# VectorE's order in a three-tap convolution loop: both outer taps ahead of an earlier chunk's product, in a fused three-network kernel

## The chip, the cores and the metric

The kernel runs on one core of one Trainium2 chip. The metric is the device time of one execution in microseconds (us), as the median of several runs. TensorE does matrix products, ScalarE activations and copies, VectorE elementwise work, GpSimd some small arithmetic, and SyncE issues the transfers.

## The reference, cut to what matters

Three networks run one after the other in float32. The first is an attention with features that are products of two sketches, the second a Fourier mixing with a normalised two-layer network, the third a network with a convolution of three taps along the sequence. The change is in the third:

```python
def _moe2_ref(x, w_in, conv_w, w_out):          # x: 4 x 1088 x 128, w_in: 128 x 1024
    h = np.maximum(x @ w_in, 0.0)
    hp = ...                                     # h with one row of zeros at either end
    conv_out = np.zeros_like(h)
    for k in range(3):
        conv_out += conv_w[k][None, None, :] * hp[:, k:k + S, :]
    gate = 1.0 / (1.0 + np.exp(-conv_out))
    return (h * gate @ w_out).astype(np.float32)
```

## The kernel before, in words

The last network's tiles lie in SBUF with the channels on the 128 partitions and the tokens along the free dimension. The last network is cut into NI = 32 chunks: chunk i is batch i // 8 and hidden channels (i % 8) * 128 and the following 127, over all 1088 tokens. There is no scheduler. Each engine's program is written out by hand and engines wait for each other through counting semaphores, so the order in the code is the order on the engine.

One chunk i passes through these steps:

- TensorE, `hidden(i, t)`: the hidden values in three pieces of 364 tokens, each as three matmuls (L519, L520, L521) of high and low parts.
- ScalarE, `relu(i)` (L790): three pieces into `h2`, a ring of HIDDENS = 5 tiles. It waits until the product of chunk i - 5, the last reader of its tile, is done.
- ScalarE, `middle_tap(i)` (L798): the middle tap times `h2` into `gate`, a ring of GATES = 9 tiles, from chunk 3 on. For the first three chunks VectorE does this (`opening_tap`, L1034).
- VectorE, `left_tap(i)` (L1043) and `right_tap(i)` (L1048): each adds its tap times shifted `h2` to `gate`, in place. The right tap waits for `left_ready`, the left tap's semaphore.
- ScalarE, `sigmoid(i)` (L803), in place, released by the right tap.
- VectorE, `product(i)` (L1055): `h2` times `gate`, in place. The last two chunks are done in three pieces each, one after the other.
- TensorE, `project(i)` (L598): three pieces, accumulated over the 8 chunks of a batch; each leaves two records in the trace, so six a chunk. After a batch's last chunk ScalarE copies the sums (L811) and SyncE stores them.

TensorE's loop does `hidden(i)`, then pieces of the second network that are left (`slots_a`, L519 to L521, and L559), then the projections of chunks 6 to 8 behind (`LAGS`), of 4 behind from chunk 30 on. After the last hidden matmuls it does the projections of chunks 27 to 31 in a row. ScalarE's loop does `relu(i + 1)`, `middle_tap(i + 1)`, `sigmoid(i - 1)`. VectorE's loop does left tap i, product i - 2 and right tap i, with low parts of the second network's results (L982, L969) in between at a few places, where `slots_a` and `slots_b` have any.

All of these tiles except TensorE's inputs lie in one large tensor, `arena`, so most rows name that tensor.

Of the kernel before, what the change touches and what calls it, by code (L numbers as in the profile page):

```python
# [70 lines left out]
NI = B * (D2 // 128)  # L71
# [39 lines left out]
def build(nc, kT_d, qT_d, v_d, s_d, ident_d, chan_d, cos_d, sin_d, w1_d, w2_d, win_d, wout_d, cw_d, out_d):  # L111
    with ExitStack() as ctx:
# [157 lines left out]
        def has_low(n):  # L270
            return n < LOW_UNTIL
# [30 lines left out]
        def token_views(x2, r):  # L302
            for side in range(2):
                turned = ps[:, bank_x2(r), side * BP * TQ:(side + 1) * BP * TQ]
                (_, b0, j0), (_, b1, j1) = UNITS[r][side * BP:(side + 1) * BP]
                if b0 != b1:
                    rows, (_, columns) = token_range(j0, side)
                    yield turned.rearrange("p (b t) -> p b t", t=TQ)[:, :, rows], x2[:, b0:b1 + 1, columns]
                elif side == 1:
                    for k in range(2):  # L310
                        rows, (_, columns) = token_range(j0 + k, side)
                        yield turned[:, k * TQ + rows.start:k * TQ + rows.stop], x2[:, b0, columns]
                else:
                    first, step = (1, 1) if j0 in LOW else (1 + S // 2, -1)
                    yield (turned.rearrange("p (j t) -> p t j", t=TQ),
                           x2[:, b0, first:first + step * 2 * TQ:step].rearrange("p (t j) -> p t j", j=2))

        def slots_a(i):
            return range(slots_before(2 * i), slots_before(2 * i + 1))

        def slots_b(i):
            return range(slots_before(2 * i + 1), slots_before(2 * i + 2))
# [519 lines left out]
        def _(dve):  # L842
# [91 lines left out]
            def mixed_rows(r):  # L934

                q, j = divmod(r, NJ)
                dve.wait_ge(cosine_done, r + 1)
                dve.wait_ge(sine_ready, r + 1)
                if r >= 1:
                    dve.wait_ge(u_ready, 4 * r)  # L940
                cosine = ps[0:TQ, SUM_BANK, 0:NS].rearrange("p (b l) -> p b l", l=L)
                for k, op in ((0, ALU.subtract), (1, ALU.add)):
                    dve.tensor_tensor(spec[:, k], cosine, sine[:], op).then_inc(spec_ready, 1)
                dve.wait_ge(spec_ready, 2 * (r + 1))
                for side in range(2):
                    for half_ in range(2):
                        x = x_nat[:, q * BP:(q + 1) * BP, side * NJ + j, half_ * 64:half_ * 64 + 64]
                        dve.tensor_tensor(x, x, spec[:, side ^ half_, :, half_:half_ + 64], ALU.add).then_inc(u_ready, 1)

            def moments(r):  # L950
                dve.wait_ge(u_ready, 4 * ROWS_OF[r])
                if r >= 1:
                    dve.wait_ge(mv_ready, r)
                for m, u in enumerate(normalised(TURN_ORDER[r])):
                    ins = dve.bn_stats(stats[:, m, :], u)
                ins.then_inc(stats_ready, 1)
                dve.wait_ge(stats_ready, r + 1)
                if r >= 3:
                    dve.wait_ge(rstd_ready, r - 2)
                for m in range(2 * BP):  # L960
                    ins = dve.bn_aggr(mv[:, r % 3, m, :], stats[:, m, :])
                ins.then_inc(mv_ready, 1)

            def normed_low(r):
                dve.wait_ge(unhi_ready, r + 1)
                if 2 <= r < RING:
                    dve.wait_ge(w1_done, C1 * (r - 1))
                high, low = turned(r)
                dve.tensor_tensor(low, ps[:, bank_turned(r), 0:G1], high.bitcast(F32),  # L969
                                  ALU.subtract).then_inc(unlo_ready, 1)  # L970

            def hidden_low(n):
                dve.wait_ge(h1hi_ready, n + 1)
                if n >= 3:
                    dve.wait_ge(w2_done, n - 2)
                dve.scalar_tensor_tensor(out=h1lo[:, n % 3, :], in0=ps[:, bank_h1(n), 0:G1], scalar=0.0,  # L976
                                         in1=h1hi[:, n % 3, :].bitcast(F32), op0=ALU.max, op1=ALU.subtract).then_inc(h1lo_ready, 1)

            def mixed_low(r):
                dve.wait_ge(x2hi_ready, written(r))  # L980
                for (turned, tokens), (_, high) in zip(token_views(x2lo, r), token_views(x2hi, r)):
                    dve.tensor_tensor(tokens, turned, high.bitcast(F32), ALU.subtract).then_inc(x2lo_ready, 1)  # L982

            def slot(n):
                r, c = divmod(n, C1)
                if n < NC1 and has_low(n):
                    hidden_low(n)
                if n in MIXED_AT:
                    mixed_rows(MIXED_AT[n])
                if c == 1 and r >= NJ:  # L990
                    mixed_low(r - 1)
                if n in MOMENTS_AT:
                    moments(MOMENTS_AT[n])
                if c == 2 and 1 <= r < NJ:
                    mixed_low(r - 1)
                if n in TURNS_AT:
                    normed_low(TURNS_AT[n])
# [39 lines left out]
            def left_tap(i):  # L1037
                if i < OPENING:
                    opening_tap(i)
                    dve.wait_ge(opening_ready, i + 1)  # L1040
                else:
                    dve.wait_ge(mid_ready, i - OPENING + 1)
                dve.scalar_tensor_tensor(out=gate[:, i % GATES, 1:S + 1], in0=h2[:, i % HIDDENS, 0:S], scalar=taps[:, i % C2, 0:1],  # L1043
                                         in1=gate[:, i % GATES, 1:S + 1], op0=ALU.mult, op1=ALU.add).then_inc(left_ready, 1)

            def right_tap(i):
                dve.wait_ge(left_ready, i + 1)
                dve.scalar_tensor_tensor(out=gate[:, i % GATES, 1:S + 1], in0=h2[:, i % HIDDENS, 2:S + 2], scalar=taps[:, i % C2, 2:3],  # L1048
                                         in1=gate[:, i % GATES, 1:S + 1], op0=ALU.mult, op1=ALU.add).then_inc(conv_ready, 1)

            def product(i):
                dve.wait_ge(gate_ready, i + 1)
                cuts = [1 + t * TT for t in range(NT)] if i >= SPLIT_FROM else [1]
                for a, z in zip(cuts, cuts[1:] + [S + 1]):
                    dve.tensor_tensor(gate[:, i % GATES, a:z], h2[:, i % HIDDENS, a:z], gate[:, i % GATES, a:z],  # L1055
                                      ALU.mult).then_inc(prod_ready, 1)
# [6 lines left out]
            for i in range(NI + 2):  # L1063
                if i < NI:
                    left_tap(i)
                if i + 1 == LAST_TURN:
                    normed_low(NR - 1)
                for n in slots_a(i + 1):
                    slot(n)
                if i >= 2:  # L1070
                    product(i - 2)
                if i < NI:
                    right_tap(i)
                for n in slots_b(i + 1):
                    slot(n)

# [93 lines left out]
```

## Time and profile before

| what | before |
|---|---|
| median of 3 runs | 259.62 us (259.18, 259.62 and 291.54) |
| profiled execution, its own time | 258.77 us |
| span of the profiled execution | 256.9 us |
| TensorE matmuls busy | 247.5 us, 96% |
| VectorE busy | 221.8 us, 86% |
| ScalarE busy | 183.8 us, 72% |
| TensorE's granted clock | 1.00 |

The span is that of the instructions on the core; the execution's own time is 1.87 us longer. Busy times overlap, so they don't add up. The chunk loop of the last network runs from about 119 us to the end. Starts are counted from the start of the span. On VectorE an instruction may start before the record of the one ahead has ended, so what one takes of the engine is read from start to start.

### The profile page before, as it was taken

How to read it: one execution, taken by the hardware profiler on the slowest of the kernel's cores; microseconds unless marked ns; L12 is line 12 of the kernel's file. 1: busy time of each engine (PE TensorE's matmuls, PEld its weight loads, DVE VectorE, ACT ScalarE, POOL GpSimd, SP SyncE). 2: the span in 40 equal slices, each digit the busy share in tenths (PEclk: the TensorE clock that was granted, in tenths of full speed). 3: DMA queues.
4: the chain of work that ended last, by engine and by line, in shares of the span. 5: the costliest groups of instructions: out<-in, count | busy, mean ns of one | idle time of the engine just before them, and what ended most of it. 6: DMA issues, size and time to landing. Idle time of an engine off the chain costs nothing.

```text
span 256.9 us, 4304 instructions
## 1 busy us (share of the span) xinstructions
PE 247.5 (96%) x1522; PEld 210.2 (82%) x1522; DVE 221.8 (86%) x395; ACT 183.8 (72%) x354; POOL 26.5 (10%) x90
## 2 busy tenths in 40 slices
PE   8999999989999999989999999999999999999985
PEld 7999998989989999878876878787778777787752
DVE  0846978997998779897999999989979999998992
ACT  2342427333486455878999998979999999978872
POOL 0000000002603333474000000000000000000000
PEclk9999999999999999999999999999999999999999
DMA  7959630300000000000000000002000002002002
GB/s 235 396 181 378 268 97 1 95 4 0 3 0 3 1 1 3 0 3 3 0 0 3 0 0 0 3 1 87 0 0 3 0 0 88 3 1 87 0 0 87
DMA packets 4341, 13.04 MB, mean 51 GB/s; under 512 B 736, under 2 KB 1504, under 8 KB 4320
## 3 DMA queue, kind: packets, MB, share of 16 engines
q1 hardware_dynamic: 4176, 12.74, 13.5%
q8 instruction: 12, 0.20, 0.3%
q14 instruction: 9, 0.07, 0.1%
q10 hardware_dynamic: 144, 0.03, 0.1%
HBM read 10.54 MB, written 2.23 MB: 50 GB/s over the span
## 4 chain that ended last, share of the span: by engine, by line
PE 48%; ACT 5%; issue 1%; DVE 1%; ACTq 0%
PE ps L598 22%; PE ps L519 7%; PE ps L521 7%; PE ps L520 7%; PE ps L559 5%; ACT arena L790 1%; ACT arena L803 1%; ACT arena L720 1%; ACT arena L798 1%; DVE arena L1043 1%; DVE arena L1055 0%; PE ps L529 0%; PE ps L550 0%; ACT x2hi L739 0%; ACT arena L811 0%
## 5 line engine op out<-in xcount | busy, mean ns | idle before, releaser
L598 PE MATMUL ps<-arena,wout 128*128 128x364 f32 (+1 forms) x192 | 62.8, 468 | 0.7 <-DVE arena L1055 0.7
L598 PEld LDWEIGHTS ps<-arena,wout 128*128 128x128 f32 x192 | 35.9, 189 | 20.8 <-issue 2.8
L790 ACT ACTIVATE arena<-ps 128x364 f32<-128x364 f32 x96 | 41.1, 491 | 4.5 <-PE ps L521 4.0
L1043 DVE SCALAR_TENSOR_TENSOR arena<-arena,taps 128x1088 f32<-128x1088 f32 x32 | 43.2, 1351 | 0.3 <-ACT arena L798 0.2
L1048 DVE SCALAR_TENSOR_TENSOR arena<-arena,taps 128x1088 f32<-128x1088 f32 x32 | 43.2, 1351 | 0.1
L1055 DVE TENSOR_TENSOR arena<-arena 128x1088 f32<-128x1088 f32 (+2 forms) x36 | 41.5, 1164 | 1.4 <-ACT arena L803 1.2
L519 PE MATMUL ps<-x2hi,wlo 128*128 128x364 f32 x96 | 39.4, 411 | 0.9 <-ACT arena L790 0.7
L803 ACT ACTIVATE arena<-arena 128x1088 f32<-128x1088 f32 x32 | 35.8, 1121 | 1.9 <-DVE arena L1048 1.9
L798 ACT ACTIVATE arena<-arena,taps 128x1088 f32<-128x1088 f32 x29 | 35.4, 1221 | 0.6
L520 PE MATMUL ps<-x2lo,whi 128*128 128x364 f32 x96 | 31.5, 328 | 0.0
L521 PE MATMUL ps<-x2hi,whi 128*128 128x364 f32 x96 | 31.5, 328 | 0.0
L848 DVE TENSOR_TENSOR arena<-arena 109x1280 f32<-109x1280 f32 (+1 forms) x12 | 21.9, 1843 | 6.1 <-ACT arena L671 6.0
L519 PEld LDWEIGHTS ps<-x2hi,wlo 128*128 128x128 f32 x96 | 18.0, 188 | 6.8 <-ACT arena L790 3.2
L520 PEld LDWEIGHTS ps<-x2lo,whi 128*128 128x128 f32 x96 | 18.1, 188 | 3.3 <-issue 1.2
L671 ACT ACTIVATE arena<-ps 109x320 f32<-109x320 f32 (+2 forms) x16 | 6.7, 425 | 18.0 <-PE ps L434 15.6
L446 PE MATMUL ps<-arena 121*128 121x66 f32 x144 | 18.6, 270 | 0.0
L720 ACT ACTIVATE arena<-x_nat,arena 109x128 f32<-109x128 f32 x40 | 16.4, 483 | 2.6 <-POOL arena L402 2.6
L976 DVE SCALAR_TENSOR_TENSOR h1lo<-ps,h1hi 128x436 fp32r<-128x436 f32 x22 | 13.3, 605 | 5.5 <-ACT h1hi L734 5.5
L521 PEld LDWEIGHTS ps<-x2hi,whi 128*128 128x128 f32 x96 | 18.1, 188 | 0.0
L446 PEld LDWEIGHTS ps<-arena 121*128 121x128 f32 x144 | 17.7, 192 | 0.0
L679 ACT ACTIVATE arena<-ps 128x436 f32<-128x436 f32 x20 | 10.6, 536 | 9.3 <-PE ps L461 9.1
L477 PE MATMUL ps<-arena 128*109 128x66 f32 x160 | 17.1, 260 | 0.1
(90 smaller groups left out, 425.4 us busy)
## 6 DMA issues: line engine op xcount, KB each, us to landing
arena<-v_d SPq DMA_DIRECT2D x4, 594.0 KB, 3.8
arena<-qT_d SPq DMA_DIRECT2D x3, 545.0 KB, 6.3
arena<-kT_d SPq DMA_DIRECT2D x3, 544.5 KB, 5.4
out_d<-arena SPq DMA_DIRECT2D x3, 544.0 KB, 2.7
cos_t<-cos_d SPq DMA_DIRECT2D x1, 926.5 KB, 5.8
sin_t<-sin_d SPq DMA_DIRECT2D x1, 926.5 KB, 7.6
arena<-qT_d SPq DMA_DIRECT2D x2, 272.5 KB, 4.2
wraw<-w_d SPq DMA_DIRECT2D x2, 256.0 KB, 5.2
```

The source lines that it names most:

```text
L446: mm = pe.matmul(ps[:, KV_BANK, pair * 2 * V1:(pair + 1) * 2 * V1], kphi[:, b % 2, t, 2 * pair:2 * pair + 2, :].rearrange("p h f -> p (h f)"),
L519: pe.matmul(out, lo, rhi, start=first, stop=False)
L520: pe.matmul(out, hi, rlo, start=False, stop=False)
L521: return pe.matmul(out, hi, rhi, start=False, stop=last)
L598: pe.matmul(ps[:, OUT_BANK + t, 0:z - a], wout[:, c, :], gate[:, i % GATES, a:z], start=(c == 0), stop=(c == C2 - 1)).then_inc(wout_done, 1)
L790: act.activation(h2[:, i % HIDDENS, t * TT:(t + 1) * TT], ps[:, bank_p(n), 0:TT], ACT.Relu).then_inc(h2_ready, 1)
L798: act.activation(gate[:, i % GATES, 1:S + 1], h2[:, i % HIDDENS, 1:S + 1], ACT.Copy, scale=taps[:, i % C2, 1:2]).then_inc(mid_ready, 1)
L803: act.activation(gate[:, i % GATES, 1:S + 1], gate[:, i % GATES, 1:S + 1], ACT.Sigmoid).then_inc(gate_ready, 1)
L848: dve.tensor_tensor(phi.rearrange("p t h (i j) -> p (t h) i j", j=R), a, c, ALU.mult).then_inc(ready, 1)
L1043: dve.scalar_tensor_tensor(out=gate[:, i % GATES, 1:S + 1], in0=h2[:, i % HIDDENS, 0:S], scalar=taps[:, i % C2, 0:1], in1=gate[:, i % GATE ...
L1048: dve.scalar_tensor_tensor(out=gate[:, i % GATES, 1:S + 1], in0=h2[:, i % HIDDENS, 2:S + 2], scalar=taps[:, i % C2, 2:3], in1=gate[:, i % ...
L1055: dve.tensor_tensor(gate[:, i % GATES, a:z], h2[:, i % HIDDENS, a:z], gate[:, i % GATES, a:z], ALU.mult).then_inc(prod_ready, 1)
```

## The change

In every pass of VectorE's loop `right_tap(i)` comes directly behind the left tap (and behind what the second network still has there), and `product(i - 2)` behind both. The other engines' programs are the same, and so are all waits and tiles.

```diff
                 for n in slots_a(i + 1):
                     slot(n)
+                if i < NI:
+                    right_tap(i)
                 if i >= 2:
                     product(i - 2)
-                if i < NI:
-                    right_tap(i)
                 for n in slots_b(i + 1):
                     slot(n)
```

VectorE, the passes of chunks 2 and 3, before. L1043 is a left tap, L1055 a product (of chunks 0 and 1 here), L1048 a right tap, L969 a low part of the second network; `arena` holds `gate` and `h2`:

```order
L1043 SCALAR_TENSOR_TENSOR arena<-arena,taps 128x1088 [waits opening_ready]
L969 TENSOR_TENSOR late_lo<-ps,late_hi 128x436 [waits unhi_ready]
L1055 TENSOR_TENSOR arena<-arena 128x1088 [waits gate_ready]
L1048 SCALAR_TENSOR_TENSOR arena<-arena,taps 128x1088 [waits left_ready]
L1043 SCALAR_TENSOR_TENSOR arena<-arena,taps 128x1088 [waits mid_ready]
L1055 TENSOR_TENSOR arena<-arena 128x1088 [waits gate_ready]
L1048 SCALAR_TENSOR_TENSOR arena<-arena,taps 128x1088 [waits left_ready]
```

The same place with the change:

```order
L1043 SCALAR_TENSOR_TENSOR arena<-arena,taps 128x1088 [waits opening_ready]
L969 TENSOR_TENSOR late_lo<-ps,late_hi 128x436 [waits unhi_ready]
L1048 SCALAR_TENSOR_TENSOR arena<-arena,taps 128x1088 [waits left_ready]
L1055 TENSOR_TENSOR arena<-arena 128x1088 [waits gate_ready]
L1043 SCALAR_TENSOR_TENSOR arena<-arena,taps 128x1088 [waits mid_ready]
L1048 SCALAR_TENSOR_TENSOR arena<-arena,taps 128x1088 [waits left_ready]
L1055 TENSOR_TENSOR arena<-arena 128x1088 [waits gate_ready]
```

The right tap of chunk 2 still has L969 between itself and its left tap; that of chunk 3, as most behind it, follows its left tap directly.

VectorE at the end of the program, the last two passes with taps (chunks 30 and 31, products 28 and 29) and then product 30 in three pieces, before:

```order
L1043 SCALAR_TENSOR_TENSOR arena<-arena,taps 128x1088 [waits mid_ready]
L1055 TENSOR_TENSOR arena<-arena 128x1088 [waits gate_ready]
L1048 SCALAR_TENSOR_TENSOR arena<-arena,taps 128x1088 [waits left_ready]
L1043 SCALAR_TENSOR_TENSOR arena<-arena,taps 128x1088 [waits mid_ready]
L1055 TENSOR_TENSOR arena<-arena 128x1088 [waits gate_ready]
L1048 SCALAR_TENSOR_TENSOR arena<-arena,taps 128x1088 [waits left_ready]
L1055 TENSOR_TENSOR arena<-arena 128x364 [waits gate_ready]
L1055 TENSOR_TENSOR arena<-arena 128x364
L1055 TENSOR_TENSOR arena<-arena 128x360
```

The same place with the change:

```order
L1043 SCALAR_TENSOR_TENSOR arena<-arena,taps 128x1088 [waits mid_ready]
L1048 SCALAR_TENSOR_TENSOR arena<-arena,taps 128x1088 [waits left_ready]
L1055 TENSOR_TENSOR arena<-arena 128x1088 [waits gate_ready]
L1043 SCALAR_TENSOR_TENSOR arena<-arena,taps 128x1088 [waits mid_ready]
L1048 SCALAR_TENSOR_TENSOR arena<-arena,taps 128x1088 [waits left_ready]
L1055 TENSOR_TENSOR arena<-arena 128x1088 [waits gate_ready]
L1055 TENSOR_TENSOR arena<-arena 128x364 [waits gate_ready]
L1055 TENSOR_TENSOR arena<-arena 128x364
L1055 TENSOR_TENSOR arena<-arena 128x360
```

Product 29 was the last but one of the full-length instructions, ahead of the right tap of chunk 31; now it is the last, behind it. Product 31's three pieces follow in both.

## Rows read from the trace of the kernel before

**Rows 1.** The page: busy us, share of the span, instructions of each engine.

```profile
PE 247.5 (96%) x1522; PEld 210.2 (82%) x1522; DVE 221.8 (86%) x395; ACT 183.8 (72%) x354; POOL 26.5 (10%) x90
```

**Rows 2.** Busy time by stage; behind it granted clock, DMA share, GB/s.

```profile
core 0: us, PE busy (x) PEld busy (x) DVE busy (x) ACT busy (x) POOL busy (x), PEclk, DMA share, GB/s
138.00:248.00 110.00, 109.65 (x477) 83.11 (x475) 105.41 (x94) 101.78 (x165) 0.00 (x0) 1.00 0.04 16
248.00:257.00 9.00, 5.76 (x18) 3.32 (x18) 4.27 (x8) 2.54 (x4) 0.00 (x0) 1.00 0.17 62
```

**Rows 3.** The chain that ended last, from 242 us: start us, us, what.

```profile
243.03 0.48 ACT arena L790
...
244.53 1.21 ACT arena L798
...
245.77 1.35 DVE arena L1043
247.12 1.21 DVE arena L1055
...
248.38 5.78 PE ps L598 x18
```

**Rows 4.** Timeline of TensorE at the end; in brackets idle time before, and releaser.

```profile
245.66 2.00 PE L598 MATMUL ps<-arena,wout 128*128 128x364 f32 x6
...
248.38 5.76 PE L598 MATMUL ps<-arena,wout 128*128 128x364 f32 x18 [0.72 <-DVE arena L1055]
```

**Rows 5.** Timeline of VectorE at the end.

```profile
235.56 1.29 DVE L1055 TENSOR_TENSOR arena<-arena 128x1088 f32<-128x1088 f32 x1 [1.24 <-ACT arena L803]
...
238.03 1.35 DVE L1043 SCALAR_TENSOR_TENSOR arena<-arena,taps 128x1088 f32<-128x1088 f32 x1
...
249.50 2.77 DVE L1055 TENSOR_TENSOR arena<-arena 128x364 f32<-128x364 f32 x6
```

**Rows 6.** Timeline of ScalarE: a ReLU, a middle tap, the last sigmoid.

```profile
146.67 1.18 ACT L790 ACTIVATE arena<-ps 128x364 f32<-128x364 f32 x3
...
236.65 1.21 ACT L798 ACTIVATE arena<-arena,taps 128x1088 f32<-128x1088 f32 x1
...
249.62 1.11 ACT L803 ACTIVATE arena<-arena 128x1088 f32<-128x1088 f32 x1 [1.89 <-DVE arena L1048]
```

**Rows 7.** Timeline of VectorE: the passes of chunks 0 and 1.

```profile
121.83 1.35 DVE L1043 SCALAR_TENSOR_TENSOR arena<-arena,taps 128x1088 f32<-128x1088 f32 x1
123.21 1.36 DVE L1048 SCALAR_TENSOR_TENSOR arena<-arena,taps 128x1088 f32<-128x1088 f32 x1
...
125.30 1.35 DVE L1043 SCALAR_TENSOR_TENSOR arena<-arena,taps 128x1088 f32<-128x1088 f32 x1
126.69 1.35 DVE L1048 SCALAR_TENSOR_TENSOR arena<-arena,taps 128x1088 f32<-128x1088 f32 x1
```

**Rows 8.** Timeline of VectorE: the pass of chunk 5, and its successor's start.

```profile
141.13 1.35 DVE L1043 SCALAR_TENSOR_TENSOR arena<-arena,taps 128x1088 f32<-128x1088 f32 x1
142.40 1.29 DVE L1055 TENSOR_TENSOR arena<-arena 128x1088 f32<-128x1088 f32 x1
143.60 1.35 DVE L1048 SCALAR_TENSOR_TENSOR arena<-arena,taps 128x1088 f32<-128x1088 f32 x1
144.86 1.35 DVE L1043 SCALAR_TENSOR_TENSOR arena<-arena,taps 128x1088 f32<-128x1088 f32 x1
```

**Rows 9.** Timeline of VectorE: its last two waits for ScalarE's x2hi, and left tap 22.

```profile
191.46 0.74 DVE L982 TENSOR_TENSOR x2lo<-ps,x2hi 128x218 fp32r<-128x218 f32 x3 [1.93 <-ACT x2hi L739]
...
207.47 0.75 DVE L982 TENSOR_TENSOR x2lo<-ps,x2hi 128x218 fp32r<-128x218 f32 x3 [0.35 <-ACT x2hi L739]
...
210.59 1.36 DVE L1043 SCALAR_TENSOR_TENSOR arena<-arena,taps 128x1088 f32<-128x1088 f32 x1
```

**Rows 10.** Timeline of TensorE: its first matmuls.

```profile
1.18 3.65 PE L604 MATMUL ps<-arena 128*128 128x256 f32 x8 [1.18 <-DVE arena L999]
```

## The prediction

> **What bounds the kernel now.** I read the page's busy times first, then the busy time by stage, then the chain that ended last, and last the three engines' timelines around its end. Over the whole span TensorE is busy 247.5 of 256.9 us, VectorE 221.8 [rows 1]. By stage: from 138 to 248 us TensorE is busy 109.65 of 110 us, VectorE 105.41 [rows 2]. So in the loop over the 32 chunks of the last network, where the change is, TensorE sets the pace; VectorE is the second, with about 4.6 us to spare in 110. From 248 us on TensorE has only 18 records left, 5.76 us of work, and VectorE is doing the products that feed them.
>
> The chain shows how the end is made [rows 3]. Read it forwards: the last hidden matmuls of TensorE release the ReLU of chunk 31 at 243.03; three ReLU pieces, then the middle tap (244.53, 1.21 us), then VectorE's left tap (245.77, 1.35), then one product (247.12, 1.21), then the 18 records of the last three projections (248.38, 5.78), then the output copy and store. The product on the chain is that of chunk 29, because VectorE's pass i does left tap i, product i-2, right tap i. TensorE had finished the projection of chunk 28 (started at 245.66) and waited 0.72 us for this product [rows 4]. It is the only wait of its matmuls for VectorE's products. Products 30 and 31 follow at 249.50 [rows 5], and are early enough: VectorE is through with both at 252.27, while TensorE, at 1.83 us a chunk, starts chunk 31 near 252.1 and its last piece near 253.3.
>
> **The change part by part.** Nothing is added or removed; per pass VectorE's order left, product, right becomes left, right, product. I take it in four points.
>
> (a) *The tap pair becomes directly dependent.* The right tap waits on the left tap's own semaphore and reads the tile that it has just written. In the trace this stands in the first passes, which have no product yet: 121.83 to 123.21 and 125.30 to 126.69, 1.385 us from start to start [rows 7]. With other work between, one tap starts 1.265 us before the next instruction and a product 1.20: 141.13, 142.40, 143.60, 144.86, a pass of 3.73 us [rows 8]. So the pair costs 0.12 us, and a pass becomes 1.385 + 1.265 + 1.205 = 3.855 us. Right tap to product and product to left tap do not exist in the trace; I take for them the independent starts just given, since neither reads what the other wrote. Their bounds are the shortest and the longest distances that these rows show: 1.20 to 1.39 for the first, 1.20 to 1.33 for the second (its own 1.29 and the 0.03 that the dependent pair keeps), so -0.07 to +0.25 us a pass. Of the 30 passes from chunk 2 on, four keep other work between the taps (a low part of TensorE's input or of the normed rows), so 26 pay: 26 x 0.12 = 3.1 us more of VectorE time.
>
> What hides it: VectorE's idle time in this stage. Only what has gathered since VectorE last waited matters. It waited 1.93 us at 191.46 and again at 207.47, and left tap 22 starts at 210.59 [rows 9]. From 207.47 the two orders reach that point together (two starts of 1.265 and 1.20 in either order). Then left tap 29 would be ready at 210.59 + 7 x 3.855 = 237.57, but its middle tap ends at 236.65 + 1.21 = 237.86 [rows 6], so it starts near 237.9 (238.03 before). Two passes on, left tap 31 could start at 237.9 + 7.71 = 245.61; it starts at 245.77 as before, since the middle tap of chunk 31 ends only then. So the 3.1 us cost nothing at the end: all is absorbed. The 1.24 us that VectorE waits for the sigmoid of chunk 26 at 235.56 [rows 5] goes, because the right tap fills it; it buys nothing, as VectorE then waits for the middle taps instead.
>
> Without that cover: the cover ends when left tap 31 is later than 245.77. Two passes after 237.9 leave (245.77 - 237.9)/2 = 3.935 us a pass, so a pair could cost 0.20 us before anything moves; at 0.3 us it would be 2 x 0.10 from there, and left tap 29 itself would come at 210.59 + 7 x 4.03 = 238.8, 0.9 late: 1.1 us in all.
>
> The Trainium skill, "VectorE: DVE Perf Modes", section "The DRAIN you can't avoid", says that a semaphore between consecutive VectorE operations costs nothing extra, since the pipe is flushed after each anyway. The rows of this trace differ, 1.385 against 1.265. By the page the sum below would be 0.12 us smaller, as one pair lies on the final chain.
>
> (b) *Every product comes later by a right tap, some 1.26 us plus what has gathered.* Who waits for products: TensorE's projections and ScalarE's ReLU of the chunk five later, which takes over the product's buffer. The tightest of these ReLUs is that of chunk 8, at 146.67 [rows 6]. Product 3 comes after left tap 5, which goes from 141.13 to 141.38 (two slower passes): right tap 142.77, product 144.03 to 145.32. That leaves 1.35 us. All other ReLUs have more. The projections run six to eight chunks behind the hidden matmuls, down to four at the end. There, product 28 stands behind left tap 30 (241.75) and right tap 30 (243.13): 244.40 to 245.69, where TensorE wanted it at 245.66 [rows 4]. That is 0.1 us of waiting, swallowed by the next point. Cost of (b) in the loop: nothing.
>
> (c) *The end.* Product 29 now stands behind right tap 31. Left tap 31 at 245.77, right tap 31 at 247.15, product 29 at 248.42, ending at 249.71; TensorE begins 0.06 us after that, at 249.77, where it began at 248.38. From there its 18 records run unbroken if products 30 and 31 are in time: they run 249.62 to 252.39, and the last piece is wanted near 254.7. What follows (output copy, store) is unchanged. So the end moves by 249.77 - 248.38 = 1.39 us, in effect the whole start-to-start time of a right tap.
>
> (d) *What becomes earlier.* Every right tap, so every sigmoid may start up to 1.2 us sooner. ScalarE waited for a right tap only once in this stage, 1.89 us at 249.62 for the last one [rows 6]; all its other sigmoids found theirs done, so nothing is gained in the loop. The last sigmoid would start near 248.5, which lets product 31 start at once; but it was not late before.
>
> **The sum.** 0 (a) + 0 (b) + 1.39 (c) - 0 (d): the span goes from 256.9 to 258.3 us, the profiled execution from 258.77 to 260.16. The times shown are 259.18, 259.62 and 291.54, the median 259.62; the two near each other and the profiled one have 259.18 in their middle, and 259.18 + 1.39 = 260.57. I forecast 260.6 us.
>
> **The rivals.**
>
> *VectorE becomes the bound.* If the pair, or right tap to product, costs 0.3 us and not 0.12, left tap 31 is 1.1 us late and the end moves by 1.39 + 1.1 + 0.2 = 2.7 us: 261.9. At 0.4 the 1.35 us before the ReLU of chunk 8 begin to go as well, and ScalarE would hold TensorE earlier in the loop. Against it: the pairs of the trace all show 1.38 or 1.39, after instructions of the same shape. 5%.
>
> *Nothing to be measured.* The right tap's 1.39 us would be hidden if left tap 31 came 1.3 us sooner. For it speaks that VectorE loses its 1.24 us wait; against it that the middle tap of chunk 31, fed by TensorE, fixes that start. Or the size drowns in the spread of the runs (0.44 us between two of before). 259.2. 9%.
>
> *Faster.* If the last sigmoid (1.11 us) and not product 29 decided the end, its earlier start would give up to 1.1 us: 258.1. The chain goes through product 29 and TensorE has work until 253 without product 31's last piece. 3%.
>
> *Slower by over 2%: TensorE's clock.* Its wait before the last 18 records grows from 0.72 us to about 2.0 (247.75 to 249.77). In this trace the granted clock is 1.00 in every slice, and no wait that TensorE is named for is longer than the 1.18 us at the start [rows 10], so a wait of 2 us is beyond what the rows show. The first matmuls, of 256 columns, took 3.65 us for 8 records, 1.78 ns a column (their row of granted clock reads 1.00, their pace does not); the 18 records of 364 columns at 0.305 us each make 0.84 ns [rows 4, 10]. At the slower pace the last projections take 5.5 x 2.1 = 11.6 us, 6.1 more: 266.7. It decides if the clock falls within a wait of 2.0 us that did not fall within 1.2. 3%.
>
> The Trainium skill, "TensorE: Matmul & The Clock Gate", section "Part 1: The HAM clock gate (the "warmup" mystery)", says that an idle array falls back to half its clock and must earn it back. The rows here show no such fall within the kernel.
>
> **How the numbers follow.** The forecast, the end moving by 1 to 2 us, has 80%; the rivals have 5, 9, 3 and 3%. The range goes from 259.2 (nothing to be measured) to 262.2 (259.62 + 1.39 + the 1.1 of a dearer pair), since the middle of the runs is itself uncertain by some 0.4 us. A measurement of this kernel can tell about 2% from no change, 5.2 us; only the clock rival, and half a percent of mishap on the other side, lie beyond: faster 0.01, within 2% 0.95, slower 0.04.
>
> **What would show it.** In the profile of the changed kernel: (a) tap to tap 1.38 us from start to start, VectorE some 3 us less idle between 130 and 248 us and its 1.24 us wait near 235 gone; (b) no ReLU waiting for a product; (c) the chain's last part is left tap, right tap, product, then 18 records, TensorE waiting about 2 us for it; (d) the last sigmoid near 248.5. I am wrong if left tap 31 starts later than its middle tap's end, if TensorE waits for VectorE or ScalarE before 245 us, or if the 18 records take more than 5.8 us.

## The result, and the profile after

The changed kernel took 262.27 us in the median of 6 runs (260.97 to 294.56), the kernel before 259.49 beside it. The ratio is 1.0103 with a 95% interval of 1.0071 to 1.0135: slower, by 2.7 us, and within 2%. The forecast was 260.6 us in a range of 259.2 to 262.2, an end later by 1.39 us. (Some executions of most of these kernels, called disturbed here, take about 30 us longer, in the one trace that holds such an execution with TensorE at about half its pace until about 73 us; medians count them, ratios leave them out.)

The profiled execution took 260.97 us with a span of 259.2, 2.3 us above that of before. The end of its chain answers to [rows 3]; start us, us, what:

```profile
243.88 0.48 ACT arena L790
...
245.38 1.21 ACT arena L798
...
246.61 1.36 DVE arena L1043
...
248.00 1.35 DVE arena L1048
249.35 1.21 DVE arena L1055
250.57 0.04 issue
250.61 5.78 PE ps L598 x18
```

From the first ReLU piece of chunk 31 to the first of the 18 last records it is now 250.61 - 243.88 = 6.73 us, before 248.38 - 243.03 = 5.35. The right tap (L1048) has entered the chain, and the end costs 1.38 us more. The same at TensorE, with the wait in brackets, to be held against [rows 4]:

```profile
244.67 4.03 PE L598 MATMUL ps<-arena,wout 128*128 128x364 f32 x12
250.61 5.77 PE L598 MATMUL ps<-arena,wout 128*128 128x364 f32 x18 [1.91 <-DVE arena L1055]
```

The other 0.85 us of the span lie ahead of the change: the ReLU of chunk 31 itself stands at 243.88 and not at 243.03, and that lead is there from the start. ScalarE's first copy of the sketches, in a part of the program that is the same in both, begins at 6.71 us here (the first of these rows) and began at 5.87 before (the second), 0.84 us earlier:

```profile
6.71 0.44 ACT L671 ACTIVATE arena<-ps 121x320 f32<-121x320 f32 x1 [4.06 <-PE ps L434]
```
```profile
5.87 0.44 ACT L671 ACTIVATE arena<-ps 121x320 f32<-121x320 f32 x1 [3.21 <-PE ps L434]
```

That leaves a puzzle. The profiled execution, once its late start is taken off, has just the forecast 1.4 us. But it is the fastest of the changed kernel's; the other undisturbed ones took 261.67 to 262.55 us. Their record has one more number that differs: a mean granted clock of TensorE of 0.993, where the profiled one has 0.999 (its clock is lower only after 258.9 us, behind the last matmul) and all undisturbed runs of the kernel before have 1.000.

VectorE in the loop, the passes of chunks 3 and 4 after; it answers to [rows 8]:

```profile
134.52 1.35 DVE L1043 SCALAR_TENSOR_TENSOR arena<-arena,taps 128x1088 f32<-128x1088 f32 x1
135.90 1.36 DVE L1048 SCALAR_TENSOR_TENSOR arena<-arena,taps 128x1088 f32<-128x1088 f32 x1
137.17 1.29 DVE L1055 TENSOR_TENSOR arena<-arena 128x1088 f32<-128x1088 f32 x1
138.37 1.35 DVE L1043 SCALAR_TENSOR_TENSOR arena<-arena,taps 128x1088 f32<-128x1088 f32 x1
```

Tap to tap 1.38, right tap to product 1.27, product to left tap 1.20: a pass of 3.85 us, as worked out. The busy time by stage (PE, PEld, DVE, ACT, POOL, granted clock, DMA share, GB/s), against [rows 2]:

```profile
138.00:248.00 110.00, 110.00 (x481) 83.76 (x480) 107.45 (x94) 102.03 (x167) 0.00 (x0) 1.00 0.04 16
```

VectorE's idle time in this stage shrank from 4.59 to 2.55 us and TensorE lost none. From 130 us on it shrank by 2.0 us as well, where the prediction had some 3: part of the 0.12 us of a pair stands in the trace as a short gap ahead of the right tap, and all 32 of these gaps come to 1.0 us where they were 0.1. The 1.24 us wait of VectorE near 235 is gone, as forecast.

### The profile page after: what moved, and what is told of

It is laid out like the page before. It is cut to its first block, busy times and chain, and to the rows that moved or that the text cites. A ratio compares the mean times of both kernels' runs of the same rounds, so it can differ in the third digit from the quotient of the medians.

```text
span 259.2 us, 4304 instructions
## 1 busy us (share of the span) xinstructions
PE 248.5 (96%) x1522; PEld 210.9 (81%) x1522; DVE 223.9 (86%) x395; ACT 183.8 (71%) x354; POOL 26.6 (10%) x90
## 4 chain that ended last, share of the span: by engine, by line
PE 47%; ACT 6%; DVE 2%; issue 1%; ACTq 0%
PE ps L598 21%; PE ps L519 7%; PE ps L521 7%; PE ps L520 7%; PE ps L559 5%; ACT arena L790 2%; ACT arena L803 1%; ACT arena L798 1%; ACT arena L720 1%; DVE arena L1043 1%; DVE arena L1048 1%; DVE arena L1055 0%; PE ps L529 0%; PE ps L550 0%; ACT x2hi L739 0%
## 5 line engine op out<-in xcount | busy, mean ns | idle before, releaser
L1048 DVE SCALAR_TENSOR_TENSOR arena<-arena,taps 128x1088 f32<-128x1088 f32 x32 | 43.3, 1352 | 1.0
L1043 DVE SCALAR_TENSOR_TENSOR arena<-arena,taps 128x1088 f32<-128x1088 f32 x32 | 43.1, 1348 | 0.4 <-ACT arena L798 0.2
L1055 DVE TENSOR_TENSOR arena<-arena 128x1088 f32<-128x1088 f32 (+2 forms) x36 | 41.3, 1160 | 0.0
L434 PE MATMUL ps<-sketch,arena 128*109 128x64 f32 (+1 forms) x152 | 17.5, 270 | 0.0
```

## The experiments

Ratios are to the kernel before, run beside them. Experiments 1, 2, 7 and the first of 3 ran on one chip, 4, 5, 6 and the first of 8 on a second, the repeats of 3 and 8 on a third. Line numbers of some kernels are a few higher, since lines were added.

**1. The changed kernel again (after_again).** No edit.

> The changed kernel once more, unaltered. What is open: its profiled execution took 260.97 us, 2.2 more than that of before, of which 0.85 us were there already at 120 us, ahead of the change's place, and its other executions took 261.7 to 262.6. Theory 'end': the last product is 1.39 us later, and the rest is a varying start of the kernel (the first matmuls run at the slow pace for a longer or shorter while), which the kernel before shares; then the median stands 1.4 us above before, the ratio 1.005 to 1.007. Theory 'end and clock': TensorE's wait of 1.9 us ahead of the last 18 records also lowers its clock in some executions; then the ratio stays near 1.010 and the mean clock of those runs is lower than that of before.

262.45 us (262.31 to 263.11), ratio 1.0128 (1.0109 to 1.0148), mean clock 0.993 in all four executions. This time the profile holds such an execution. The end of its chain:

```profile
247.78 1.35 DVE arena L1048
249.14 1.21 DVE arena L1055
250.35 0.04 issue
250.39 7.47 PE ps L598 x18
```

The same 18 records take 7.47 us and not 5.78. Its windows of one microsecond show why; the number behind the last busy time, that of POOL, is the granted clock:

```profile
250.00:251.00 1.00, 0.61 (x2) 0.49 (x3) 1.00 (x3) 0.28 (x1) 0.00 (x0) 1.00 0.00 0
251.00:252.00 1.00, 1.00 (x4) 0.54 (x3) 1.00 (x3) 0.00 (x0) 0.00 (x0) 0.80 0.00 0
252.00:253.00 1.00, 1.00 (x3) 0.51 (x2) 1.00 (x3) 0.00 (x0) 0.00 (x0) 0.50 0.00 0
253.00:254.00 1.00, 1.00 (x3) 0.67 (x2) 0.02 (x1) 0.00 (x0) 0.00 (x0) 0.50 0.00 0
254.00:255.00 1.00, 1.00 (x3) 0.48 (x2) 0.00 (x0) 0.00 (x0) 0.00 (x0) 0.50 0.00 0
255.00:256.00 1.00, 1.00 (x5) 0.66 (x4) 0.00 (x0) 0.00 (x0) 0.00 (x0) 0.99 0.00 0
```

The granted clock is 0.50, the lower level of 1.2 GHz, from about 251.6 (the mean of 0.80 in the second row) to 255.0, with three records a microsecond instead of five. The records lose half of those 3.4 us, and 7.47 - 5.78 = 1.69 us is what is measured. "End and clock" it is: 1.4 + 1.7 = 3.1 us, a ratio of 1.012.

**2. The new order except in the last pass (all_but_last).**

```diff
-                if i >= 2:
-                    product(i - 2)
-                if i < NI:
-                    right_tap(i)
+                if i < NI - 1:
+                    right_tap(i)
+                if i >= 2:
+                    product(i - 2)
+                if i == NI - 1:
+                    right_tap(i)
```

> The new order in the passes of chunks 2 to 30; in the last pass with taps (chunk 31) the old one, product 29 ahead of right tap 31. Theory 'end': nothing of the cost lies in the loop, so the time is that of before, ratio 0.999 to 1.001, the 26 dearer tap pairs absorbed. Rival 'backlog': the dearer pairs and later products cost something in the loop; then 0.5 to 1.4 us stay, ratio 1.002 to 1.005.

259.62 us, ratio 0.9998 (0.9984 to 1.0012), clock 1.000. Its chain ends as before, 248.84 - 243.50 = 5.34 us from ReLU to records:

```profile
243.50 0.48 ACT arena L790
...
246.23 1.35 DVE arena L1043
247.58 1.21 DVE arena L1055
248.80 0.04 issue
248.84 5.78 PE ps L598 x18
```

So 29 of the 30 swapped passes are free, within the 0.4 us of the interval, though 25 of them cost VectorE 0.12 us each (the 26 of the full change without the pair of chunk 31). "Backlog" falls.

**3. The swap in the last pass alone (only_last, only_last_b).** The mirror image: `right_tap` ahead of the product only where i == NI - 1.

> The old order everywhere but in the last pass (chunk 31), where right tap 31 stands ahead of product 29. Theory 'end': the whole cost, 1.39 us in the span from this one swap, ratio as that of the full change. Rival 'backlog': only a part of it.

261.88 us, ratio 1.0105 (1.0088 to 1.0123), mean clock 0.993 in all five. One swap makes the whole loss. It stood 0.57 us under experiment 1, so I ran both again side by side:

> The swap in the last pass alone, again. Theory 'end and clock' with a start that varies: as the full change beside it. Rival 'backlog': 0.5 us below it.

> The changed kernel again, beside the swap in the last pass alone, since in the earlier runs the two stood 0.6 us apart (262.45 and 261.88) though the ends of both traces last alike from the last ReLU to the last record. Theory 'end and clock' with a start that varies: both the same here, ratio 1.010 to 1.013, intervals overlapping by more than half. Rival 'backlog': the full change is again 0.5 us above the swap alone.

The swap alone: 1.0110 (1.0083 to 1.0137). The full change: 1.0101 (1.0071 to 1.0130), from two undisturbed executions of 262.06 and 261.57 us, both at 0.993. The difference of the first pair did not come back; what is left of it, 0.2 us the other way, is within the intervals. Of the six executions of the swap alone five had 0.993, and one, the profiled one, 1.000 at 260.96 us. Its last lines are those of the first profile above almost to the hundredth:

```profile
244.67 3.83 PE L598 MATMUL ps<-arena,wout 128*128 128x364 f32 x12
250.61 5.77 PE L598 MATMUL ps<-arena,wout 128*128 128x364 f32 x18 [2.11 <-DVE arena L1055]
```

A wait of 2.11 us, and no lower clock in that execution. So the fall is not certain. By the mean clock it came in 10 of 11 undisturbed executions of the full change and in 10 of 11 of the swap alone.

**4. TensorE kept busy in its wait (after_fill).** On the changed kernel, in `project` of TensorE:

```diff
+                if i == NI - 3:
+                    claim(bank_p(NT * NI - 4), (h2_ready, NT * NI))
+                    for _ in range(10):
+                        pe.matmul(ps[:, bank_p(NT * NI - 4), 0:TT], whi[:, 2 * D1:2 * D1 + 128],
+                                  x2hi[:, B - 1, 0:TT], start=True, stop=True)
```

> The changed kernel, and TensorE gets ten matmuls of 364 columns (0.167 us each by the hidden matmuls' pace, 1.7 us) ahead of the projection of chunk 29; they write a PSUM bank that nobody reads any more, so no result changes. TensorE would only wait in that time. Theory 'end and clock': the clock stays at 1.00 to the end, the last 18 records take 5.8 us as in the kernel before, and of the 3.3 us that the changed kernel costs only the 1.39 of the late product stay: ratio 1.005 to 1.007. Rival (the clock falls for another reason, or falls with the wait for a product whatever TensorE does): ratio stays at 1.011 to 1.014, records 7.5 us.

260.17 us (260.04 to 260.93), ratio 1.0049 (1.0035 to 1.0062), clock 1.000 in all six. TensorE's end:

```profile
243.94 4.03 PE L603 MATMUL ps<-arena,wout 128*128 128x364 f32 x12
247.53 2.07 PE L596 MATMUL ps<-x2hi,whi 128*128 128x364 f32 x10
249.89 5.77 PE L603 MATMUL ps<-arena,wout 128*128 128x364 f32 x18 [0.28 <-DVE arena L1060]
```

Ten matmuls whose results nobody reads make the kernel 1.4 to 2.0 us faster than the plain change, by the ratios of 1.0103 and 1.0128 against 1.0049. The product still ends at the same place (249.89 - 243.15 = 6.74 us behind the ReLU), so what is left, 1.27 us by the ratio, is the late product, and what went is the clock. That splits the loss in two by measurement. The plain changed kernel did not run on this chip. That the clock falls here too after a wait of 1.88 us shows in experiment 6, but in two executions of five and not in ten of eleven, so six without a fall say less than the two counts side by side suggest.

**5. A shorter wait (after_split29).** On the changed kernel:

```diff
-SPLIT_FROM = NI - 2
+SPLIT_FROM = NI - 3
```

> The changed kernel with product 29 in three pieces (SPLIT_FROM = NI - 3). TensorE may start after the first, near 248.95 and not 249.77, so its wait shrinks from 2.0 to 1.2 us. VectorE's products follow one another here, with no right tap between, so TensorE is not held again. Theory 'end and clock', if 1.2 us is short enough: clock 1.00, 0.6 us above before, ratio 1.002 to 1.003. If 1.2 us is already too long: clock 0.993 and 2.3 us above before, ratio 1.009. Theory 'end' alone: ratio 0.003 under that of the changed kernel, 1.010.

260.01 us, ratio 1.0024 (1.0010 to 1.0037), mean clock 0.999 or 1.000 in all its executions. Its trace is of an execution of 292.22 us, of which the surplus lies ahead of the chunk loop; the end reads:

```profile
281.85 5.77 PE L598 MATMUL ps<-arena,wout 128*128 128x364 f32 x18 [1.17 <-DVE arena L1055]
```

TensorE waits 1.17 us, and the last records keep their clock. By the ratio 0.6 us are left of the loss: the clock's part is gone, and half of the late product's.

**6. The pair made dearer (pair_dear).** On experiment 2, with its harmless last pass (`gap` is a new tile of one column, `gap_done` a new semaphore):

```diff
             def right_tap(i):
                 dve.wait_ge(left_ready, i + 1)
+                if 2 <= i < NI - 1:
+                    dve.memset(gap[:], 0.0).then_inc(gap_done, 1)
+                    dve.wait_ge(gap_done, i - 1)
```

> The new order in the passes of chunks 2 to 30 and the old one in chunk 31, which cost nothing; and between the two taps of every pass from 2 to 30 a memset of one column that waits for the left tap, and that the right tap waits for. The pair is then dearer by another 0.15 to 0.25 us, a pass about 4.05. By the working of the prediction the loop can hide a pair of 0.20 us and no more: with a pass of 4.05 left tap 29 comes at 210.59 + 7 x 4.05 = 238.9 and left tap 31 near 247.0, 1.3 us late. Theory 'end and clock': TensorE's wait grows from 0.7 to 2.0 us, and the clock falls here too, though the last pass has the old order: 1.3 + 1.7 = 3.0 us, ratio 1.011 to 1.013. Theory 'end' without the clock: ratio 1.005. If VectorE's reserve is larger than worked out: ratio under 1.002.

261.79 us, ratio 1.0096 (1.0067 to 1.0124). The undisturbed executions were two of 262.39 us at 0.993, and three of 260.61 to 261.20 at 0.999 or 1.000. The ratio lies between the two that were forecast (1.005 without the clock, 1.011 to 1.013 with it), since only some executions lost their clock. One pass of its VectorE, left tap 31, and TensorE's end:

```profile
237.86 0.06 DVE L1051 MEMSET gap<- 128x1 f32 x1
237.95 1.35 DVE L1053 SCALAR_TENSOR_TENSOR arena<-arena,taps 128x1088 f32<-128x1088 f32 x1
...
241.84 0.06 DVE L1051 MEMSET gap<- 128x1 f32 x1
...
248.39 1.35 DVE L1045 SCALAR_TENSOR_TENSOR arena<-arena,taps 128x1088 f32<-128x1088 f32 x1
```
```profile
248.53 9.29 PE L600 MATMUL ps<-arena,wout 128*128 128x364 f32 x24 [1.88 <-DVE arena L1060]
```

A pass is 241.84 - 237.86 = 3.98 us, 0.07 less than I expected. Left tap 31 comes 248.39 - 243.81 = 4.58 us after the first ReLU piece of its chunk (at 243.81), before 2.74: 1.84 us late, where I had 1.3. The working had VectorE start even at 207.47, but here its last low parts began at 209.30, 1.05 us late when the 0.78 us of this execution's late start are taken off: the backlog reaches further back. TensorE waits 1.88 us, this time already for product 28. So VectorE's reserve ends between a pass of 3.855 us (nothing lost) and one of 3.98, and the clock falls here too, in two executions of five, although the last pass has the old order: it goes with the wait and not with the swap.

**7. Product 29 in pieces in the old order (split29).** The edit of experiment 5, on the kernel before.

> The kernel before with product 29 in three pieces as 30 and 31 are (SPLIT_FROM = NI - 3), so that TensorE can start its projection after the first third. If the 0.72 us wait of TensorE at 248.38 is what the end is made of, it goes nearly away: the first piece ends near 247.6, so 0.6 to 0.7 us faster, 258.8, ratio 0.997 to 0.998, if three pieces cost VectorE no more than 0.2 us. If TensorE then waits for products 30 and 31 instead, the gain is under 0.3 us.

259.34 us, ratio 0.9996 (0.9984 to 1.0008). TensorE starts chunk 29 without a wait and then stands 0.50 us for the first piece of product 30, behind right tap 31:

```profile
247.96 1.34 DVE arena L1055 x3
249.30 1.26 DVE arena L1048
250.56 0.46 DVE arena L1055
251.02 0.04 issue
251.07 3.95 PE ps L598 x12
```

That is the second of the two cases expected: the 0.72 us wait of [rows 4] only moves by one chunk, as 0.50 us. VectorE has no spare time at the end.

**8. Product 29 ahead of left tap 31 (early29, early29b).** ScalarE does sigmoid 29 ahead of middle tap 31, VectorE product 29 ahead of left tap 31 (both leave their old places, which is not printed here):

```diff
+                    if i + 1 == NI - 1:
+                        sigmoid(i - 1)
                     if i + 1 >= OPENING:
                         middle_tap(i + 1)
...
+                if i == NI - 1:
+                    product(i - 2)
                 if i < NI:
                     left_tap(i)
```

> The old order, but ScalarE does sigmoid 29 ahead of middle tap 31, and VectorE product 29 ahead of left tap 31. Product 29 then ends near 247.0, before TensorE is through with chunk 28 (247.65); left tap 31 comes 1.1 us later (246.9), right tap 31 248.25, and the first piece of product 30 is ready near 250.0, where TensorE wants it at 249.5. The 0.72 us wait becomes one of 0.5, and the end comes 0.4 to 0.5 us sooner: ratio 0.998. If product 31 (sigmoid 31 from 249.6 to 250.7) comes too late instead, nothing or a loss of up to 0.5 us.

259.27 us, ratio 0.9997 (0.9986 to 1.0008), where 0.998 was expected: in the trace TensorE still waits 0.49 us for the first third of product 30, and the 0.2 us that its last record gains can't be told from nothing. Then that third was also moved ahead of right tap 31:

> As early29 (sigmoid 29 ahead of middle tap 31, product 29 ahead of left tap 31), and the first third of product 30 between left tap 31 and right tap 31. early29 still had TensorE wait 0.49 us, for that third, which stood behind the right tap. Worked out from its trace: the third is ready near 248.6 and TensorE goes on from chunk 29 without a wait at 249.5; the second third, behind the right tap, near 250.3 (wanted at 250.1), product 31's first near 251.5 (wanted at 251.4). TensorE's last records end near 253.4, 0.7 us sooner than in the kernel before: ratio 0.997. If right tap 31 and with it sigmoid 31 come too late instead (0.5 us later than in early29), the gain is 0.2 us or less, ratio 0.999 to 1.000.

258.74 us, ratio 0.9981 (0.9966 to 0.9996), 0.5 us faster than the kernel before, where 0.7 was expected; its interval only just leaves out no change. It is the only version that beats both kernels. TensorE's end, 20 records in a row, then a wait of 0.20:

```profile
243.83 6.28 PE L598 MATMUL ps<-arena,wout 128*128 128x364 f32 x20
250.31 3.37 PE L598 MATMUL ps<-arena,wout 128*128 128x364 f32 x10 [0.20 <-DVE arena L1057]
```

## Why the prediction was right on the late product and wrong to leave out the clock

- **(a) The dearer pair, absorbed.** Right. The pair measures 1.38 us, the pass 3.85, and experiment 2 loses nothing. Left tap 29 starts at 238.74 and left tap 31 at 246.61, with the late start of 0.85 us taken off at 237.89 and 245.76, where 237.9 and 245.77 were worked out. Both unmeasured distances came out at the value taken. The rule of the Trainium skill, "VectorE: DVE Perf Modes", section "The DRAIN you can't avoid", that a semaphore between operations costs nothing extra does not hold for this pair, with 1.38 against 1.26 us; what else than the semaphore could make the difference (the second operation reads what the first wrote) was not tried apart. The end of the reserve, put at a pass of 3.935 us, lies between 3.855 and 3.98. But the working of what happens beyond it was too kind: it started VectorE fresh at 207.47.
- **(b) Later products in the loop.** Right: ScalarE's ReLUs wait only for TensorE, as before, and the records of chunks 27 and 28 take 4.03 us instead of 3.83, the forecast 0.1 us being 0.2.
- **(c) The end, 1.39 us.** Right: 1.38 in the chain, 1.27 by experiment 4.
- **(d) Earlier sigmoids.** Right. The last one begins at 249.39, or 248.5 with the late start taken off, and helps nobody.
- **The rival "TensorE's clock", and what failed.** This was the step that was wrong: the sum put the clock at nothing. The rival named the right place and cause, gave them 3%, and priced them at 6.1 us, for all 18 records at the slow pace. The runs say: 10 of 11 executions, and 1.69 us, since the low clock lasts 3.4 us and the rest runs at full pace. What the prediction had on it, that no wait of TensorE in the trace is longer than 1.18 us, was no evidence on a wait of 2.0, as it said itself; it did not bear out a chance as low as 3%. The sum left the term out and gave 1.39 us instead of 1.39 + 0.9 x 1.69 = 2.9. So the median of 262.27 us lies 0.07 us above the upper end of the range, 262.2. That it comes so near is luck: that end was set by the base and by a dearer pair (1.1 us), which did not come, and not by this term. The prediction's own sign of being wrong, 18 records that take more than 5.8 us, is there in three of the five traces of the full change and of the swap alone, with 7.47. The Trainium skill, "TensorE: Matmul & The Clock Gate", section "Part 1: The HAM clock gate (the "warmup" mystery)", has the array at 1.2 GHz when it has been idle: the trace of experiment 1 agrees in the level, with a granted clock of 0.50, and in that a wait went before. But there the clock fell while the matmuls ran again.
- **The other rivals.** "Nothing to be measured" and "faster" fell. "VectorE becomes the bound" is real at a pass of 3.98 us, but the change, at 3.855, stays under it.
- **The start.** The forecast took the middle of the runs of before for its base, and that was sound: their undisturbed runs spread over 1.2 us (258.55 to 259.75). The traces of before and after, one of each, differ by 0.85 us ahead of the chunk loop, which is most of that.

What stays open: why one execution in eleven of either kernel kept its clock through the last records, after waits of 1.91 and 2.11 us, and three in five of experiment 6, while the others lost it, in the traces after waits of the same length. Also whether the rate of the falls hangs on the chip, and the cause of the varying start. In the profile after, TensorE puts out fewer records between 4 and 7 us (5, 7 and 10 in a microsecond) than in that of before (7, 12 and 13), as a slower clock would have it, but the granted clock reads 1.00 there in both. Nor does all of it lie so early: the third trace of the full change has its first copy at 5.88, like the kernel before, and its first middle tap on VectorE at 121.24 against 120.97.

## What to carry to other kernels

Where one engine sets the pace and another feeds it, an order that is free in 29 passes can cost its full price in the last, because in the middle TensorE takes each product several chunks later, and at the end at once: work out the last pass by itself. When the sum says that TensorE will wait longer than in any row of the profile, its clock is a term of the sum and not a footnote: price it at half pace for a few microseconds (3.4 us here, a loss of 1.7), and look whether the wait can be filled with matmuls or shortened by handing the product over in pieces. And look at the granted clock of every execution, as the profiled one may be the exception. Experiment 6 adds that spare time is not to be counted from the last wait alone when every pass gets dearer.

## What the runs showed of the hardware that was not expected

After waits of 1.88 to 2.11 us TensorE's granted clock fell to 0.50 in most executions (22 of 27 by the mean clock), and it fell not within the wait but after the matmuls had gone on. In experiment 1 the wait ended at 250.39, the clock was 1.00 up to 251 and 0.50 from about 251.6 to 255.0, although the engine was busy throughout. In the three other traces that hold a fall (only_last, after_b, pair_dear) it came some 1.4, 0.3 and 0.3 us after the wait's end, by the means of one-microsecond windows, and the low stretch was 3.4 us each time. After waits of 0.72 us (the kernel before) and 1.17 us (experiment 5) the traces show no slower record, and the mean clock of all their undisturbed executions is 0.999 or 1.000. A right tap directly behind the left tap that it needs starts 1.38 us after it, where an instruction that does not need it starts 1.26 us after, for 1088 columns; the memset of one column between two taps, with both waits, made a pass 0.12 us longer still (3.98 against 3.855).
